# Gate logits computed in column quarters of TensorE, x pieces spread over a round, maximum and column-sum hops moved

## The reference

```python
x = attention(q, k, v)                       # 4 x 8 heads, 576 positions, window 64
h = x @ w_in                                 # [2304, 512] @ [512, 2048]
x = where(h > 0, h, exp(min(h, 0)) - 1) @ w_out
logits = x @ w_gate                          # [2304, 512] @ [512, 8]
P = exp(logits - logits.max())
for _ in range(8):                           # Sinkhorn
    P /= P.sum(1, keepdims=True) + 1e-9
    P /= P.sum(0, keepdims=True) + 1e-9
    P *= 2304 / 8
out = sum(P[:, e:e+1] * (relu(x @ w1[e]) @ w2[e]) for e in range(8))
```

## Time and profile before

| | us |
|---|---|
| median of 3 runs (lowest, highest) | 1946.71 (1944.76, 1950.9) |
| the profiled execution | 1947.36 |
| its span in the trace | 1945.6 |
| TensorE busy | 1898.2 (98%) |
| VectorE busy | 1528.0 (79%) |
| ScalarE busy | 849.8 (44%) |
| mean granted TensorE clock, share of full | 0.993 |

### The profile page before, as it was taken

How to read it: one execution, slowest core, us unless ns; L and a number is a source line. 1 busy time by engine, 2 the same in 40 slices (tenths; PEclk the granted TensorE clock), 3 DMA queues, 4 the chain that set the end, 5 groups by cost and what they waited for, 6 DMA issues and landing times.

```text
span 1945.6 us, 31304 instructions
## 1 busy us (share of the span) xinstructions
PE 1898.2 (98%) x11640; PEld 1866.3 (96%) x11640; DVE 1528.0 (79%) x1839; ACT 849.8 (44%) x1401; POOL 649.7 (33%) x511
## 2 busy tenths in 40 slices
PE   8879999999989999999999999999999999999998
PEld 6569999999989999999999999999999999999998
DVE  6977878777878788787787787787877877877877
ACT  7767655555555342342433333433433333433422
POOL 5643332332232334233323234233333233243320
PEclk9999999999999999999999999999999999999999
DMA  9874666663456566666576666666665666666654
GB/s 256 270 277 168 227 206 215 205 215 134 169 181 220 202 227 222 216 225 224 193 252 212 214 213 220 216 209 220 221 235 200 235 215 209 220 222 215 204 192 146
DMA packets 96709, 414.73 MB, mean 213 GB/s; under 512 B 9776, under 2 KB 10800, under 8 KB 96560
## 3 DMA queue, kind: packets, MB, share of 16 engines
q1 hardware_dynamic: 96560, 412.74, 62.4%
HBM read 374.88 MB, written 37.82 MB: 212 GB/s over the span
## 4 chain that ended last, share of the span: by engine, by line
PE 90%; DVE 5%; issue 3%; ACT 1%; POOL 0%; ACTq 0%; DVEq 0%; POOLq 0%
PE ps L1229 29%; PE ps L1231 29%; PE ps L1233 29%; PE ps L1191 1%; PE ps L1288 1%; PE ps L1217 1%; PE ps L1207 1%; DVE xs L868 1%; DVE scratch L876 1%; DVE yacc L1007 1%; DVE ss L905 0%; DVE scratch L882 0%; DVE hb L933 0%; ACT ss L732 0%; DVE hb L980 0%
## 5 line engine op out<-in xcount | busy, mean ns | idle before, releaser
L732 ACT ACTIVATE ss<-hb 128x768 fp32r<-128x768 f32 x420 | 347.3, 843 | 597.9 <-DVE hb L987 282.7
L1229 PE MATMUL ps<-ss,w2t 128*128 128x384 f32 x1680 | 573.2, 341 | 6.7 <-DVE yacc L1007 5.6
L1229 PE MATMUL ps<-xs,w1t 128*128 128x384 f32 x1680 | 567.9, 338 | 7.4 <-DVE hb L980 5.6
L1231 PE MATMUL ps<-ss,w2t 128*128 128x384 f32 x1680 | 571.9, 340 | 0.0
L1233 PE MATMUL ps<-ss,w2t 128*128 128x384 f32 x1680 | 571.8, 340 | 0.0
L1231 PE MATMUL ps<-xs,w1t 128*128 128x384 f32 x1680 | 565.6, 337 | 0.0
L1233 PE MATMUL ps<-xs,w1t 128*128 128x384 f32 x1680 | 565.2, 336 | 0.0
L1007 DVE TENSOR_TENSOR yacc<-ps,yacc 128x768 f32<-128x768 f32 x396 | 377.9, 954 | 191.4 <-PE ps L1233 183.6
L905 DVE TENSOR_TENSOR ss<-hb,ss 128x768 fp32r<-128x768 f32 x420 | 399.5, 955 | 24.2 <-ACT ss L732 14.3
L556 POOL TENSOR_TENSOR w1t<-wraw,w1t 128x512 fp32r<-128x512 f32 x140 | 188.0, 1355 | 510.9 <-DVE ss L905 321.4
L556 POOL TENSOR_TENSOR w2t<-wraw,w2t 128x512 fp32r<-128x512 f32 x140 | 182.8, 1322 | 434.5 <-DVE hb L928 235.2
(11 more groups left out here) (92 smaller groups left out, 1337.2 us busy)
## 6 DMA issues: line engine op xcount, KB each, us to landing
xs<-x_store SPq DMA_DIRECT2D x388, 768.0 KB, 4.3
wraw<-moe_w_dram SPq DMA_DIRECT2D x32, 1024.0 KB, 7.1
x_store<-xs SPq DMA_DIRECT2D x32, 768.0 KB, 4.1
pb<-p_store SPq DMA_DIRECT2D x24, 384.0 KB, 3.9
x_store<-w2t SPq DMA_DIRECT2D x10, 768.0 KB, 3.9
scratch<-q_dram SPq DMA_DIRECT2D x16, 288.0 KB, 4.7
scratch<-k_dram SPq DMA_DIRECT2D x16, 288.0 KB, 7.3
scratch<-v_dram SPq DMA_DIRECT2D x16, 288.0 KB, 7.3
```

Of the source, the lines that this page charges most:

```text
L732: nc.scalar.activation(ss[:, step, 0, :], hq(r, HOME[step]), ACT.Copy).then_inc(s_hi_done, 1)
L1229: nc.tensor.matmul(bank, w_parts[:, step, 0, cols], hi, start=step in FRESH and kt == 0, stop=False, skip_group_check=True)
L1231: nc.tensor.matmul(bank, w_parts[:, step, 0, cols], lo, start=False, stop=False, skip_group_check=True)
```

## The change

Three things are changed; the arithmetic of the products stays.

1. The gate product is spread over steps 1 to 4 of rounds 11 to 13. In steps 1, 2 and 3 two token tiles of 96 are done with `wg` (padded to 32 columns) as weights and 96 columns of `yacc` moving, each of the four k tiles into its own quarter of 32 array columns (L1339 of the changed kernel), which leaves four partial sums in four partition quarters. ACT moves them to `logit_parts` (L718), and in the next step two matmuls against `adder` sum the quarters (L1331); ACT or DVE moves the sums to `gate` (L721, L1091). The last two of the eight tiles are done the old way in step 1 (L1348). In steps 2 to 4 TensorE waits for `parts_placed`. The hop now stands behind the seventh matmul of the up product, not behind the sixth.
2. The tables of the x pieces give other places: sums 0 and 1 in step 3 (was 4), sum 2 in step 0 of the next round (was 6), sum 3 in step 1 (was 0); pieces 3 to 6 in steps 1, 2, 3, 4 of the next round (were 6, then 0, 2, 3). In round 0 `add_c` of step 5 comes ahead of `act_f` 1.
3. The turn of the maximum goes to (13,5), its spread to (14,0), the exponential to (14,1), the first rows to (14,2). Hops are at (14,3), (14,5), (15,1), (15,3), (15,5), (16,1), (16,3), (16,5), and P_HOP at (17,0).

```diff
-        for at, step in ((3, 0), (4, 1), (6, 2), (6, 3)):
+        for at, step in ((3, 0), (4, 1), (6, 2)):
             XPREP[w][at].append((cc, step))
-        for at, step in ((0, 4), (2, 5), (3, 6)):
+        for at, step in ((1, 3), (2, 4), (3, 5), (4, 6)):
             XPREP[w + 1][at].append((cc, step))
-        XSUMS[0 if cc < CHUNKS else w][0 if cc < CHUNKS else 4] = [(cc, 0), (cc, 1)]
-        XSUMS[w][6] = [(cc, 2)]
-        XSUMS[w + 1][0] = [(cc, 3)]
+        XSUMS[0 if cc < CHUNKS else w][0 if cc < CHUNKS else 3] = [(cc, 0), (cc, 1)]
+        XSUMS[w + 1][0] = [(cc, 2)]
+        XSUMS[w + 1][1] = [(cc, 3)]
...
-    SINK_HOPS = [(MAX_WINDOW, 4), (MAX_WINDOW, 6), (MAX_WINDOW + 1, 1), (MAX_WINDOW + 1, 3), (MAX_WINDOW + 1, 5),
-                 (MAX_WINDOW + 2, 0), (MAX_WINDOW + 2, 2), (MAX_WINDOW + 2, 4)]
-    P_HOP = (SCALE_WINDOW - 2, 6)
+    SINK_HOPS = [(MAX_WINDOW, 3), (MAX_WINDOW, 5)]
+    SINK_HOPS += [(MAX_WINDOW + 1 + i // 3, 1 + 2 * (i % 3)) for i in range(SINKHORN_STEPS - 2)]
+    P_HOP = (SCALE_WINDOW - 1, 0)
...
+            def move_parts(w, step):
+                nc.scalar.activation(logit_parts[:], c_spare(w, step, HT, HT + TT), ACT.Copy).then_inc(parts_placed, 1)
+
+            def move_logits(w, step, first, at):
+                nc.scalar.activation(tiles(w, first), c_spare(w, step, HT + at, HT + at + E)[0:TT], ACT.Copy) \
+                    .then_inc(logits_moved, 1)
+
+            def gate_work(w, step):
+                if not GATE_WINDOW <= w < MAX_WINDOW:
+                    return
+                act.wait_ge(c_done, STEPS * w + step + 1)
+                if step == 1:
+                    move_logits(w, step, CHUNK_TILES - 2, TT + E)
+                else:
+                    move_logits(w, step, 2 * (step - 2), TT)
+                move_parts(w, step)
...
                     relu(r, 0)
                     hi(r, 0)
                 x_piece(1)
+                if w == MAX_WINDOW:
+                    act.wait_ge(shift_placed, 1)
+                    nc.scalar.activation(gate[:], gate[:], ACT.Exp, bias=gate_shift[0:TT, :]).then_inc(gate_exped, 1)
+                gate_work(w, 1)
                 weights(2)
...
             def product(banks, step, w_parts, place, x_parts, done, between=None):
                 for j in range(2):
-                    if j == 1 and between is not None:
-                        between()
...
                         nc.tensor.matmul(bank, w_parts[:, step, 0, cols], hi, start=step in FRESH and kt == 0,
                                          stop=False, skip_group_check=True)
+                        if j == 1 and kt == 0 and between is not None:
+                            between()
...
-                if step in (2, 4) and GATE_WINDOW <= w < MAX_WINDOW:
+                if 1 <= step <= 4 and GATE_WINDOW <= w < MAX_WINDOW:
                     c1 = w - GATE_WINDOW
...
+                        wait_y(pe, FF_ROUNDS - CHUNKS + c1, 6)
+                    if step >= 2:
+                        pe.wait_ge(parts_placed, 3 * c1 + step - 1)
+                        at = HT + TT + (E if step == 4 else 0)
+                        for j in range(2):
+                            nc.tensor.matmul(spare(w, step, j, at, at + E)[0:TT, :], logit_parts[:, j, :], adder[:],
+                                             start=False, stop=True, skip_group_check=True)
+                    if step <= 3:
+                        for j in range(2):
+                            first = c1 * CT + (2 * (step - 1) + j) * TT
+                            for kt in range(KT):
+                                quarter = slice(kt * P // KT, (kt + 1) * P // KT)
+                                nc.tensor.matmul(spare(w, step, j, HT, HT + TT)[quarter, :], wg[:, kt, :],
+                                                 yacc[:, kt, first:first + TT], start=False, stop=True,
+                                                 skip_group_check=True)
...
-                if w == MAX_WINDOW and step == 0:
+                if w == MAX_WINDOW - 1 and step == 5:
                     pe.wait_ge(token_maxed, 1)
...
-                if w == MAX_WINDOW and step == 2:
+                if w == MAX_WINDOW and step == 0:
                     pe.wait_ge(all_maxed, 1)
```

More of the change, by code:

```diff
@@ L142, in build_program @@
         ones = sb("ones", [P, P])
-        wg = sb("wg", [P, KT, E])
+        wg = sb("wg", [P, KT, P // KT])
+        adder = sb("adder", [P, E])
         gate = sb("gate", [TT, E, TILES])
@@ L294, in build_program @@
         y_copied = sem("y_copied")
-        logits_done = sem("logits_done")
+        parts_placed = sem("parts_placed")
+        logits_moved = sem("logits_moved")
         logits_placed = sem("logits_placed")
@@ L701, in snap, with tiles @@
                 nc.scalar.activation(pair2(hq(r, quarter)), c_banks(r, step), ACT.Copy).then_inc(c_snap, 1)
+            def tiles(w, first):
+                t = (w - GATE_WINDOW) * CHUNK_TILES + first
+                return gate[:, :, t:t + 2].rearrange("p e t -> p t e")
+            def move_parts(w, step):
[12 more added lines that the diff above has]
+                move_parts(w, step)
             def snap_p1(r):
@@ L1126, in _ @@
                     add_y(before, 1)
+                gate_work(w, 2)
+                if down:
                     add_y(before, 2)
@@ L1139, in _ @@
                 gate_work(w, 4)
+                if w == 0:
+                    add_c(r, 5, 3, H21)
                 if up:
@@ L1148, in _ @@
                 if up:
-                    add_c(r, 5, 3, H21)
+                    if w > 0:
+                        add_c(r, 5, 3, H21)
                     gate_work(w, 5)
@@ L1279, in hop @@
             def hop(w, step):
-                if step in (2, 4) and GATE_WINDOW <= w < MAX_WINDOW:
+                if 1 <= step <= 4 and GATE_WINDOW <= w < MAX_WINDOW:
                     c1 = w - GATE_WINDOW
-                    pe.wait_ge(gate_loaded, 16)
-                    wait_y(pe, FF_ROUNDS - CHUNKS + c1, 6)
-                    first = 0 if step == 2 else CHUNK_TILES // 2
-                    for t in range(first, first + CHUNK_TILES // 2):
-                        for kt in range(KT):
-                            nc.tensor.matmul(spare(w, step, 0, HT + t * E, HT + (t + 1) * E)[0:TT, :],
-                                             yacc[:, kt, c1 * CT + t * TT:c1 * CT + (t + 1) * TT], wg[:, kt, :],
-                                             start=False, stop=kt == KT - 1, skip_group_check=True)
@@ new lines, in hop @@
+                    if step == 1:
+                        for j in range(2):
+                            first = c1 * CT + (CHUNK_TILES - 2 + j) * TT
+                            at = HT + TT + E
+                            for kt in range(KT):
+                                nc.tensor.matmul(spare(w, step, j, at, at + E)[0:TT, :], yacc[:, kt, first:first + TT],
+                                                 wg[:, kt, 0:E], start=False, stop=kt == KT - 1, skip_group_check=True)
+                if w == MAX_WINDOW - 1 and step == 5:
@@ L1315, in hop_read @@
                     pe.wait_ge(logits_placed, w - GATE_WINDOW + 1)
+                if w == MAX_WINDOW and step == 0:
+                    pe.wait_ge(all_maxed, 1)
                 if w == MAX_WINDOW and step == 2:
-                    pe.wait_ge(all_maxed, 1)
-                if w == MAX_WINDOW and step == 4:
                     pe.wait_ge(shift_placed, 1)
```

62 lines of the change are left out of this document (35 added, 27 removed).

## The result

| | before | after |
|---|---|---|
| median of the runs, us | 1948.81 (4 runs, 1944.76 to 1951.05) | 1928.06 (4 runs, 1926.15 to 1930.83) |
| the profiled execution, us | 1947.36 | 1927.98 |
| its span in the trace, us | 1945.6 | 1926.1 |

The ratio of the times is 0.9897, with a 95% interval of 0.9874 to 0.992.

What follows compares the result with a forecast made beforehand. TensorE, busy 98% of the span, was taken to bound the kernel. Terms -1.6 + 5.1 - 2.3 - 1.1 - 2.5 - 0.7 - 3.7 - 3.4 = -10.2 gave 1937 us, 8-in-10 range 1929 to 1946.

Steps and rivals of the forecast that it cites:

- Nothing else is on the path.: Closing claim: `adder` and clearing `wg` fall before the first score, P at (17,0) is ready in time; no further term.
- Part 1, gate matmuls: Rounds 11 to 13: gate products fall from 15.4 to 13.8 us, quarter matmuls at 0.083 each; gain 1.6.
- the 0.43: Idle of weight loads at two shape changes, 0.26 and 0.17 us; full cost per hop if mode changes drain the engine.
- Part 2, the wait for the parts: TensorE waits for ACT's `logit_parts` in step 1: 2.5 us in round 11, 1.3 each in 12 and 13; loss 5.1.
- Part 3, x pieces: New x tables and round 0 order shorten waits: gains 2.3 in round 12, 1.1 in round 2, 2.5 in round 0.
- an up product for an x piece: Sign: an up product waiting for an x piece in rounds 12 to 14 would make the forecast too low.
- Part 4, the Sinkhorn hops: Moved hops: round 14 waits 4.2 for 4.91, gain 0.7; the 3.68 wait in round 16 goes, gain 3.7.
- The rival that (16,5) would wait: Columns at (16,3) meet GpSimd's weight sums, so 3.7 and 3.4 stay: 1944; counted within the no-change rival, chance 0.24.
- Part 5, the clock: Two low clock stretches around 642.5 go with their wait, gain 3.4; four remain in rounds 11 to 14.
- side by side and the clock holds: Rival: quarter matmuls at 0.04 give 3.0 more, three low stretches in rounds 11 to 13 go, 5.1: 1928.5; chance 0.16.

Runs made afterwards that it cites:

- e2: The changed kernel with a pad of 32 bytes in front of `ss` and `hb`, so `ss` starts 32 past a multiple of 64; 1944.51 us, ratio 0.9975.
- e1: The kernel before with only a pad of 32 bytes ahead of `ss` and `hb`, so `ss` starts on a multiple of 64; 1937.76 us, ratio 0.994.
- e4: The changed kernel with the old gate product (16 matmuls in steps 2 and 4) and x sums 0 and 1 in step 4; 1926.61 us, ratio 0.9895.
- e5: The changed kernel with the old tables of x pieces and sums, round 0's new `add_c` order kept; 1933.05 us, ratio 0.9913.
- e14: The changed kernel with a pad ahead of `yacc`, moving all these tiles, `xs` and weights included, 32 bytes on; 1928.17 us, ratio 0.9889.
- e11: e7 with a pad of 128 bytes behind `warm`, `ss` still on a multiple of 64; 1921.24 us, ratio 0.9851 to the kernel before.
- e15: e4 (old gate product in the changed kernel) with `ss` 128 bytes further; 1920.32 us, ratio 0.9857 to the kernel before.
- e3: The kernel before with a pad of 64 bytes, so `ss` moves but stays 32 past a multiple of 64; 1946.81 us, ratio 0.9987.
- e7: The changed kernel with ACT's moves of the step 1 parts ahead of `hi` of the same round; 1925.68 us, ratio 0.9873.
- e9: The changed kernel with `hb` alone 32 bytes past a multiple of 64, `ss` where it was; 1929.25 us, ratio 0.989.

## Why the prediction was right or wrong

**The step that failed is its last one: "Nothing else is on the path."** The prediction listed what `adder` and the clearing of `wg` do in time and not what their size does to the tiles declared behind them. `ss` came to start like `w2t` modulo 64, and the down product, half of all work, became 2.2% faster, the up product 0.9% slower. The term that the prediction put at nothing is 0.19 us a round, 11 us at the most over 60 rounds. Rounds 4 to 10 and 18 to 59, in which the change has no instruction, gave 9.1 of the 20.6 us of the table above. e2 takes the gain away and e1 gives it to the kernel before, with 32 bytes each.

**The change itself is about as large as forecast.** The rounds that it touches (0 to 3 and 11 to 17) gave 11.5 us, of which the faster pace can be none up to 11 x 0.19 = 2.1: 9.4 to 11.5, for 10.2 forecast. Against the trace of e1, whose down product is as fast as that of after, the same rounds are 10.9 shorter. The terms:

- *Part 1, gate matmuls (-1.6).* A quarter matmul costs 59 ns, for 83 taken. A step with a hop is longer than a plain one of 4.18 by 2.06, 1.17, 0.93 and 0.36 in round 11 (the wait left out), 4.5 a round for 4.3. Three rounds make 13.6. Counted in the same way the old gate product took 6.94 - 4.21 = 2.73 a step, 16.4 in all and not 15.4, so the gain is 2.8. The rule of the Trainium skill, TensorEngine Tiling (Array Packing), Tiling Modes, that a change of mode drains the engine would by the prediction's estimate have made it 3.0 dearer. A hop with two changes, eight quarter matmuls and two adder matmuls costs 0.93 in all, and at 59 and 166 ns the ten matmuls alone are 0.80 of it, so the 0.43 does not show here.
- *Part 2, the wait for the parts (+5.1).* It is 1.90, 0.30 and 0.74: 2.9. The place and the releaser are right, the size in rounds 12 and 13 was too high. With part 1 it comes to nothing, and e4 confirms that.
- *Part 3, x pieces (-5.9).* Round 0 with the start of round 1: the wait is 2.63, and 2.3 us are gained for 2.5. Rounds 2 and 3: piece 3 is late by 1.87, 1.8 was said, but a low stretch of the clock (0.50 from 184.7) followed that wait and a wait of 0.67 stands in round 3; the two rounds became 0.5 longer, for 1.1 shorter. Round 12: 1.49 stayed at `act_f` 3, where the prediction had none, and 1.93 at `add_y` 6, where it had 1.5; 3.42 for 3.84 before. Two new waits of 0.45 (an up product for an x piece, which the prediction named as a sign) and 0.43 take that away, so nothing is left of the 2.3. DVE's own list shows why `act_f` 3 was not in time: the `add_c` ahead of it started 1.0 us sooner in the round, but the `act_f` between them (the first row is before, the second after) took 1.70 us for 0.96:

```profile
476.44 0.96 DVE L980 SCALAR_TENSOR_TENSOR hb<-pb,hb 128x768 f32<-128x768 f32 x1 [1.34 <-ACT pb L749]
...
473.24 1.70 DVE L1017 SCALAR_TENSOR_TENSOR hb<-pb,hb 128x768 f32<-128x768 f32 x1 [1.05 <-ACT pb L780]
```

- *The x pieces again, in e5.* The old tables under the new hops lose 3 to 5 us, for 3.4 forecast. Its longer waits are at hops: 3.82 in round 12, 1.53 in round 13 where after has none, and 2.51 in round 14 for 1.53. So the tables are needed for the hops more than for themselves.
- *Part 4, the Sinkhorn hops (-4.4).* Round 14 waits 1.53 and 1.96, 3.5 in all for 4.2 forecast (the terms named there add up to 4.1), of which it had 3.1 at the first; the round gains 1.8 for 0.7. Round 16 has no wait: 3.7 as said. The rival that (16,5) would wait fell.
- *Part 5, the clock (-3.4).* Right in round 16: 1.00 there, and the round 7.2 shorter for 7.1 forecast, 0.4 of which is the hop of P that now stands in round 17. From 440 to 680 three low stretches are left, for four forecast; with the new one in round 2 it is four. Their number is not fixed by the lists: the trace of e14, with the lists of after, has three in round 12 (479.9 to 490.1) for two, and none in round 2 or at 577.

So the x pieces fell short by 2.3 in round 12 and by 1.6 in rounds 2 and 3. The wait for the parts was 2.2 too high, the gain of the gate matmuls 1.2 and that of round 14 about 1 too low, and one low stretch of 1.7 fewer was left from 440 to 680. That the sum of the terms is right is in good part luck. Of the rivals, the time of "side by side and the clock holds" was met, 1928.5, by another cause: quarters of 59 ns for 83 are 1.7 us of its 3.0, and the clock still fell in round 12.

**What stays open.** Why starts unlike modulo 64 slow the down product: the runs show the relation of `ss` and `w2t`, not a mechanism. The other engines write and read the same tiles (DVE and ACT `ss`, ACT and GpSimd the weights), and no run leaves that out; nor does any part `w1t` from `w2t`. Why the up product does not follow the relation with `xs` and `w1t`, and what its own 22 ns depend on, which moved with the place of `ss` too (e1, e11 and e15 against after). And why e3 has 2093 where before has 2121, though both are 32 past.

## What to carry to other kernels

- An edit that adds or widens a tile moves every tile declared behind it. Before a difference is put down to waits, compare the matmul count of a window in which nothing of the change runs; here x4566 against x4595 at the same clock said it at once.
- Where a kernel is bound by TensorE, try one or two pads of 32 bytes ahead of its moving tiles and look at the start of the moving tile against that of the weights loaded beside it. The pad was worth 12 us in the kernel before and 15 to 16 us in the one after, more than the planned change.
- A hop placed later can save its wait and the low stretch behind it: both counted in round 16. But a low stretch that comes or goes in one trace is no proof, since it does so between kernels with the same lists.

## What the runs showed of the hardware

- The down product, which streams a 128x384 tile from SBUF while the next 128x128 weights are loaded, took 2.8 to 3.8 ns more a matmul (2117 to 2121 for twelve, against 2075 to 2083) where the starts of its two tiles differ by 32 modulo 64 bytes; one kernel, e3, showed only 0.8 to 1.5. The up product, with two other tiles, did not follow this.
- The paces go with the distances between the tiles modulo 512 and not with their places: all tiles moved by 32 bytes gave the same 2075 and 2105 (after, e14), and `ss` moved by 512 the same 2076 and 2091 (e1, e11).
- The pace of a product is reproducible to the nanosecond for a given placement: after and e14 have 2105 and 2075 (e4 to e7 and e9 too), although their lists differ.
- Four-quarter column tiling of 32-column weights with 96 columns moving ran at 59 ns a matmul, for 166 with the operands the other way round.
